# One matmul of 384 columns for the hi of g times hi and lo of the output weights, and a sum on the way out

## The reference

```python
w = exp(weight_gen - max(weight_gen, -1)); w = w / (sum(w, -1) + 1e-09)
x_unf = x_pad[:, idx, :].reshape(B, S, K, H, group)   # 7 rows, the row itself last
out = einsum('bshk,bskhg->bshg', w, x_unf).reshape(B * S, D)
h = out @ w_in
g = maximum(0.01 * h, h)
return g @ w_out
```

## Time and profile before

| | us |
|---|---|
| median of 3 runs | 1042.38 (1042.04 to 1043.88) |
| the profiled execution | 1043.29 |
| its span, first to last instruction | 1041.5 |
| TensorE busy | 1028.6 |
| VectorE busy | 873.6 |
| ScalarE busy | 630.8 |
| GpSimd busy | 564.5 |

### The profile page before, as it was taken

The page is one execution under the profiler, slowest core; times in us unless marked ns, Lnnn a source line. Parts: engine busy times, 40 slices in busy tenths (PEclk is TensorE's granted clock), DMA queues, the critical chain, the costliest instruction groups (busy, mean ns, idle before and its releaser), DMA issues.

```text
span 1041.5 us, 36259 instructions
## 1 busy us (share of the span) xinstructions
PE 1028.6 (99%) x16467; PEld 739.2 (71%) x16467; DVE 873.6 (84%) x1110; ACT 630.8 (61%) x1332; POOL 564.5 (54%) x369
## 2 busy tenths in 40 slices
PE   8999999999999999999999999999999999999998
PEld 4566677777777777777777777677777777777776
DVE  7999899797997979889797997979989797997511
ACT  6765565665565665565665565665566565566554
POOL 0003665565665566666566566556566556556543
PEclk9999999999999999999999999999999999999999
DMA  9101213112131310213112131220313102111100
GB/s 263 64 16 32 81 35 97 35 34 80 20 97 35 88 41 14 88 36 96 35 33 66 36 97 35 67 62 5 96 35 97 35 27 72 35 36 35 35 18 17
DMA packets 67473, 57.94 MB, mean 56 GB/s; under 512 B 56252, under 2 KB 60604, under 8 KB 65336
## 3 DMA queue, kind: packets, MB, share of 16 engines
q1 hardware_dynamic: 67196, 55.35, 19.0%
q10 hardware_dynamic: 124, 0.29, 0.1%
HBM read 29.34 MB, written 12.58 MB: 40 GB/s over the span
## 4 chain that ended last, share of the span: by engine, by line
PE 90%; DVE 7%; ACT 1%; DMA 0%; issue 0%; ACTq 0%; DVEq 0%
PE h_ps L907 44%; PE out_ps L1012 23%; PE t_ps L1012 23%; DVE gl L634 2%; DVE conv L592 2%; DVE prod L585 1%; PE h_ps L1050 1%; DMA xbuf<-in_x_dram 0%; DVE wo L614 0%; DVE x_top L597 0%; ACT xs L399 0%; DVE xs L622 0%; ACT g L414 0%; ACT gh L412 0%; DVE conv L585 0%
## 5 line engine op out<-in xcount | busy, mean ns | idle before, releaser
L286 POOL TENSOR_TENSOR gl<-g,gh 128x512 f16<-128x512 f32 x360 | 562.5, 1589 | 468.6 <-ACT g L414 468.6
L412 ACT ACTIVATE gh<-h_ps 128x512 f16<-128x512 f32 x512 | 318.1, 621 | 333.0 <-PE h_ps L907 320.5
L1012 PE MATMUL out_ps<-wo,gh 64*128 64x192 f16 x3840 | 391.3, 243 | 0.0
L1012 PE MATMUL t_ps<-wo,gh 64*128 64x192 f16 x3840 | 391.2, 243 | 0.0
L907 PE MATMUL h_ps<-xT,whA 64*128 64x512 f16 x1920 | 365.1, 377 | 2.8 <-ACT g L414 2.8
L1012 PEld LDWEIGHTS out_ps<-wo,gh 64*128 64x128 f16 x3840 | 323.5, 94 | 28.2
L1012 PEld LDWEIGHTS t_ps<-wo,gh 64*128 64x128 f16 x3840 | 323.5, 94 | 0.0
L414 ACT ACTIVATE g<-h_ps 128x512 f32<-128x512 f32 x512 | 322.8, 630 | 0.0
L592 DVE TENSOR_TENSOR conv<-conv,prod 128x768 f32<-128x768 f32 x186 | 279.7, 1504 | 1.1
L634 DVE TENSOR_TENSOR gl<-g,gh 128x512 f16<-128x512 f32 x152 | 144.9, 966 | 136.1 <-ACT g L414 136.1
L1012 PE MATMUL t_ps<-wo,gl 64*128 64x192 f16 x1920 | 233.0, 243 | 0.3 <-DVE gl L634 0.3
(11 more groups left out here) (96 smaller groups left out, 617.7 us busy)
## 6 DMA issues: line engine op xcount, KB each, us to landing
xbuf<-in_x_dram SPq DMA_DIRECT2D x15, 1344.0 KB, 6.1
out_dram<-stage SPq DMA_DIRECT2D x31, 384.0 KB, 2.3
taps<-in_weight_gen_dram SPq DMA_DIRECT2D x16, 224.0 KB, 6.0
xT_again<-xT SPq DMA_DIRECT2D x29, 64.0 KB, 2.1
rawO<-in_moe_w_out_dram SPq DMA_DIRECT2D x4, 384.0 KB, 10.0
rawA<-in_moe_w_in_dram SPq DMA_DIRECT2D x2, 512.0 KB, 8.8
xbuf<-in_x_dram SPq DMA_DIRECT2D x2, 384.0 KB, 6.6
rawD<-in_moe_w_in_dram SPq DMA_DIRECT2D x1, 512.0 KB, 7.7
```

What stands on the lines that cost most here:

```text
L286: nc.gpsimd.tensor_tensor(gl[:, f % RING, :], g[:, f % RING, :], gh[:, f % RING, :], ALU.subtract).then_inc(s_gl_p, 1)
L412: nc.scalar.activation(gh[:, f % RING, :], h_ps[f % GROUP][:], ACT.Prelu, scale=SHRINK, alpha=SLOPE).then_inc(s_gh, 1)
L1012: ins = nc.tensor.matmul(out_of(m, j), a[rows, f % RING, j * P:(j + 1) * P], wo[rows, f, part, :], start=i == 0 and k < 2 and a is gh and ...
```

## The change

For tiles 2 to 30 (`wide(m)`) the two products of gh become one of 384 columns: hi and lo of `wo` for one block are read as one row of 384, and the result goes to columns 0 to 383 of the sub-tile's bank. The products with gl are as before, into columns 0 to 191. So a bank holds two sums. ScalarE copies columns 192 to 383, times the row's scale, to `stage`, and reports on a new semaphore; VectorE then reads columns 0 to 191, multiplies by the same scale and adds what ScalarE wrote. VectorE's four instructions stand in tile m+1 right after the gl of its block 3, and now they raise `s_out_free`. Tiles 0, 1 and 31 keep the old way out.

```diff
+        def wide(m):
+            return BY_PE <= m < TILES - 1
...
-            if j < 2:
-                return out_ps[:, j, 0:D]
-            return (t32_ps, t2_32_ps)[j - 2][:, 0:D]
+            return row_bank(j)[:, 0:D]
+
+        def row_bank(j):
+            return out_ps[:, j, :] if j < 2 else (t32_ps, t2_32_ps)[j - 2][:]
...  # ScalarE, copy_out
+                if wide(m):
+
+                    for j in rows_of(m):
+                        wait_row(act, m, j)
+                        nc.scalar.activation(stage[:, u, j, :], row_bank(j)[:, D:2 * D], ACT.Copy,
+                                             scale=out_scale[:, u, j:j + 1]).then_inc(s_out_part, 1)
+                    return
...  # VectorE
+            def sums(m):
+
+                if wide(m):
+                    for k, j in enumerate(rows_of(m)):
+                        dve.wait_ge(s_out_part, SUB * (m - BY_PE) + k + 1)
+                        nc.vector.scalar_tensor_tensor(stage[:, m % 2, j, :], out_of(m, j), out_scale[:, m % 2, j:j + 1],
+                                                       stage[:, m % 2, j, :], ALU.mult, ALU.add).then_inc(s_out_free, 1)
...  # tile(m)
                 one_lo(m, 3)
+                sums(m - 1)
                 if m + 1 < TILES:
                     next_rows(m)
...  # TensorE, project
-                    products = [(gh, f, part) for f in fs for part in range(2)] if with_hi else []
+
+                    products = [(gh, f, part) for f in fs for part in ((2,) if wide(m) else (0, 1))] if with_hi else []
...
-                            ins = nc.tensor.matmul(out_of(m, j), a[rows, f % RING, j * P:(j + 1) * P], wo[rows, f, part, :],
-                                                   start=i == 0 and k < 2 and a is gh and f == 0 and part == 0,
+                            if part == 2:
+                                dst, moved = row_bank(j)[:, 0:2 * D], wo[rows, f, :, :].rearrange("p a d -> p (a d)")
+                            else:
+                                dst, moved = out_of(m, j), wo[rows, f, part, :]
+                            ins = nc.tensor.matmul(dst, a[rows, f % RING, j * P:(j + 1) * P], moved,
+                                                   start=i == 0 and k < 2 and a is gh and f == 0 and part != 1,
```

More of the change, by code:

```diff
@@ L167, in dynconv_mlp @@
         s_out_free = sem("s_out_free")
+        s_out_part = sem("s_out_part")
         s_last_row = sem("s_last_row")
```

## The result

| | before | after |
|---|---|---|
| median, us | 1042.33 (4 runs) | 1060.55 (1060.41 to 1060.96, 4 runs) |
| span of the profiled execution | 1041.5 | 1058.8 |
| TensorE, VectorE busy | 1028.6, 873.6 | 1027.2, 921.8 |

A forecast was written before the change was run, and what follows sets the result against it. TensorE was taken to set the time, with VectorE close behind. Span 1041.5 - 4.3 + 27.0 = 1064.2, adjusted to a median of 1065.1 us; range 1037.5 to 1070, the forecast's own 1060 to 1073.

The forecast's parts named there:

- TensorE's gain: Output matmuls: one 384-column pair replaces two of 192, saving 0.037 us a group, 4.3 us in all.
- The sums: VectorE's four additions after f=3's gl: 0.335 us each, making out_scale 0.87 us late in odd tiles, which pay nothing.
- The carry into the even tile: Odd tile's delay passes through ScalarE's exp and g of f=3; with the next sums, out_scale is 2.20 us late.
- The lo-of-x operations are held: VectorE's lo-of-x operations beside GpSimd's gl are held like a tensor_tensor, by about 0.96 us; not in the trace.
- The fourth hold: Even tile: GpSimd's first gl of the last group comes ahead of VectorE's f=11; TensorE stalls 1.85 us more.
- in between: Rival: lo-of-x operations held, but no extra hold at f=11; even tiles cost 1.1 us each, 1052.4 us; chance 0.17.
- the stall of an even tile: TensorE's waits for VectorE's gl in each even tile behind a softmax tile: 2.06, say 2.08 us with the restart.
- VectorE's way to the gl of f=7: Even tile: three holds paid as before, gl ends at 489.49, wanted at 489.28: a stall of 0.21 us.
- the tiles: Thirteen even tiles, m=4 to 28, stall alike, 27.0 us in all; odd tiles pay nothing.
- the faster case: Rival: lo-of-x operations not held, TensorE never stalls and keeps its 4.3 us: 1038.1 us; chance 0.23.
- some 26 waits: Sign: TensorE waits for VectorE's gl, near 0.2 and 1.9 us, only in even tiles up to 28.
- Wide matmuls that bring nothing: Rival: 384-column matmuls save nothing, the fixed part not being one per pair; 4.3 us on top of any case.

The follow-up runs named there:

- the first experiment: Changed kernel with its wide matmuls but without VectorE's four sums, ScalarE copying columns 0 to 191 out, against the kernel before: 1038.6 us, ratio 0.9959.
- taps-early run: Changed kernel with the softmax's first two operations ahead of the convolution's last piece in odd tiles, against the kernel before: 1044.5 us, ratio 1.0014.
- sums-alone run: Kernel before, keeping its two 192-column matmuls, with VectorE's four sums added as in the change: 1054.0 us, ratio 1.0111 against the kernel before.
- one addition behind f=11: Changed kernel with one convolution addition moved behind VectorE's gl of f=11, against the kernel before: 1068.5 us, ratio 1.0246.
- the control: Kernel before with only the four small scale operations moved behind the gl of f=15: 1043.0 us, ratio 1.0002 against the kernel before.

## Why the prediction was right

- **Bound.** As forecast: TensorE's time is set by when VectorE delivers, and the even tiles are where it fails.
- **TensorE's gain** was 0.040 us a group (7.845 less 7.805) and not 0.037: 4.6 us for 4.3. Shown alone in the first experiment.
- **The sums** follow each other after 0.325 us (550.28, 550.61), for 0.335. Out_scale of the odd tile comes at 519.23, 1.93 us after the hidden layer's start at 517.30, where it came 1.03 us after the earlier trace rows: 0.90 late for 0.87. Odd tiles pay nothing from 5 on, as forecast.
- **The carry into the even tile** was put at 2.36 us against TensorE (2.20 and the 0.15 TensorE gained) and measured 2.22. It goes through ScalarE's exp: the exp waited 4.3 us for VectorE's subtraction where it waited 3.4, and VectorE then waited for g ahead of the gl at 549.00 for the same 1.32 us as before, so nothing of its own held it up. The taps-early run took this away, and the stall with it.
- **The lo-of-x operations are held**, the choice on which the side of the forecast hung: 1.17 and 1.26 us against 0.27 and 0.34. The longer of the two (L622, now L636) ran at 342 to 352 ns before and up to 1297 ns after. That their two inputs in SBUF are the reason, as the Trainium skill has it (GPSIMD Engine Reference, 8. Key points), fits but wasn't tested by itself. Two inputs are not needed for a hold, at any rate: the tensor_scalar of 4 elements reads one tensor and was held too (1.02 and 1.07 us against 0.17).
- **The fourth hold**, at f=11, is there in every even tile from 6 on, and the sums-alone run shows the same hold come and go with the order of two requests. Here luck played a part: GpSimd was ahead by 0.25 us (568.52 against 568.77), where my chain had 0.48. What I had 0.45 us too long in the chain (next point) ate half of that margin. Had it been twice as much, the hold would not have come, and the result would have been near the "in between" case.
- **Mis-sized: the stall of an even tile, 1.56 us and not 2.08.** The term that failed is VectorE's way to the gl of f=7. I had it end 12.68 us after the tile's start and TensorE want it at 12.47; it ended at 12.23, and there is no stall. Of the 0.45 us, 0.14 are the smaller carry, 0.17 the holds, which cost a scalar_tensor_tensor 0.9 us and not 0.96, and 0.13 the step from out_scale to the first lo of x, 0.14 us (551.77 to 551.91) where it was 0.27. From there to the end of f=11's gl the chain took 9.66 us, as forecast. It ended at 21.89, again 0.45 ahead of my 22.34. The whole stall is the lateness of this one gl (my 0.21 at f=7 was only its first part), so 2.06 became 1.61 by this account, and 1.56 in the timeline.
- **Mis-counted: the tiles.** I had 13 alike, and no stall in an odd tile. Twelve (6 to 28) stall for 1.56, 18.7 us. Tiles 2 to 4 together have 6.1 us above 7.8 a group, where the kernel before had 2.6 above its 7.845: 3.5 more, in a stretch where VectorE is busy 34.69 of 35 us (115 to 150) and whose softmax I did not follow; the odd tile 3 is among them, with a wait of 1.68 us. Together 22.2 for my 27.0. Less 4.6, that is 17.6; the spans differ by 17.3, and the 0.3 between them lies ahead of tile 2, which starts at 86.75 instead of 87.05.
- **How much the hit is worth.** The range on record, 1037.5 to 1070, holds the faster case and the slower one, so that the time lies in it says little. The forecast's own range began at 1060, 0.5 us below the result. What was right is the mechanism and the direction, to which I had given 0.70. Of the some 26 waits, near 0.2 and 1.9 us, that I named as its sign, there are twelve of 1.4 us, and in tiles 3 and 4 two of 1.7 and one of 0.14.
- **The rivals.** The faster one needed lo-of-x operations that are not held: it fell. "In between", without the fourth hold, came closest to what the sums alone did in nine of twelve tiles. Wide matmuls that bring nothing: excluded.

## What to carry to other kernels

A second engine with 13% of its time free can still be the bound: read its slack at each point of delivery, not its busy share. Work added to it is free until the tightest delivery is missed, and from there costs its lateness in every period, with whatever collisions that lateness brings. If such a change loses, look for an operation that nobody waits for and which stands ahead of one that somebody does: here one move turned 1060.6 us into 1041.1, and leaving the crowded start alone gave 1038.8.

## What the runs showed of the hardware

- VectorE and GpSimd hold each other up by the operation, in the order of asking. The hold lengthened scalar_tensor_tensor with both tensors in SBUF (0.27 to 1.17 us), tensor_tensor (0.68 to 1.65), and even tensor_scalar of 4 elements (0.17 to 1.07): some 0.9 us each, however short the operation is by itself.
- Moving an operation out from under GpSimd's need not save its hold: in the taps-early run the operations behind it were held as before. It is saved where an operation without a hold (the tensor_reduce, 0.95 us beside GpSimd's) or an idle stretch takes its place.
- After five of six idle stretches of 2.37 or 2.38 us TensorE's granted clock fell to 0.51 for some 3.4 us, which made a wait of 2.4 us cost 4.2. After the sixth, and after one of 3.49 us, it stayed at 1.00; so it did after idle stretches of 1.4 us, once in 64 us. In tile 2, where TensorE waits 2.07 or 2.08 us for ScalarE's g in ten of the eleven traces, the lower clock came within some 2 us behind it in five (the kernel before, the change, the sums alone, one addition behind f=11 and the control) and not in the other five.
